# Four early expert slots, a bare last down, and the router of nine tiles moved from TensorE to VectorE

## What is computed

```
q, k, v: (4, 8, 576, 64)       # 2304 tokens in all, d_model 512
attn = softmax(masked(q @ k.T / 8)) @ v            # heads 0-3 local, 4-7 strided
x  = attn as (2304, 512)
xn = x / sqrt(mean(x * x) + 1e-6) * rms_g
y  = (silu(xn @ w_gate) * (xn @ w_val)) @ w_out    # d_ff 1536
logits = y @ router_w + modality_bias[modality_id] # 8 experts
e_idx  = argmax(logits); gate = softmax(logits)[e_idx]
for e in range(8):
    rows = (e_idx == e)
    out[rows] = gate[rows] * (relu(y[rows] @ w1[e]) @ w2[e])   # 512 -> 1024 -> 512
```

## Time and profile before

| | us |
|---|---|
| median of 3 runs | 913.56 (911.46 to 914.18) |
| the profiled execution | 913.16 |
| its span | 911.3 |
| start of chunks 1 to 5 (evacuation of y before) | 160.9, 257.5, 359, 455.3, 535.8 |
| start of the expert part | 617.5 |
| start of up(4), the first step of the steady loop | 678.4 |

### The profile page before, as it was taken

One profiled execution on the slowest core, in us unless ns is written; L12 is line 12 of the kernel. 1 busy time (PEld: TensorE's weight loads), 2 busy tenths in 40 slices (PEclk: granted clock), 3 DMA queues, 4 the chain that ended last, 5 costly groups with the idle time before them and its releaser, 6 DMA issues.

```text
span 911.3 us, 15931 instructions
## 1 busy us (share of the span) xinstructions
PE 888.4 (97%) x5407; PEld 760.2 (83%) x5407; DVE 443.2 (49%) x1239; ACT 363.9 (40%) x935; POOL 314.2 (34%) x371
## 2 busy tenths in 40 slices
PE   9989999999999999999999999999889999999995
PEld 5667898888888888899999999998678888888884
DVE  5864555333443335422522344774674467446651
ACT  6866413545454444521221131232262345335530
POOL 2734772334323343245234323240511122211221
PEclk9989999999999999999999999999899999999998
DMA  8982212222114210211121121610846365415511
GB/s 184 278 193 78 52 52 64 76 66 75 50 43 111 61 36 25 70 35 36 47 70 35 47 70 36 231 47 36 308 162 226 133 220 187 179 69 185 202 55 36
DMA packets 74486, 94.95 MB, mean 104 GB/s; under 512 B 38701, under 2 KB 42797, under 8 KB 74416
## 3 DMA queue, kind: packets, MB, share of 16 engines
q1 hardware_dynamic: 70656, 82.51, 29.8%
q0 software_dynamic: 3760, 11.54, 3.7%
HBM read 84.59 MB, written 10.22 MB: 104 GB/s over the span
## 4 chain that ended last, share of the span: by engine, by line
PE 91%; DVE 3%; issue 2%; POOL 1%; ACT 1%; DMA 1%; SPq 0%; ACTq 0%; DVEq 0%; POOLq 0%
PE ps L1130 34%; PE ps L1169 16%; PE ps L1621 12%; PE ps L1636 12%; PE ps L1061 3%; PE ps L1090 3%; PE ps L1071 2%; PE ps L1206 2%; PE ps L1037 2%; PE ps L1648 2%; PE ps L1199 1%; PE ps L587 1%; PE ps L1189 1%; DMA w_raw<-in_moe_w 1%; DVE w_lo L1785 1%
## 5 line engine op out<-in xcount | busy, mean ns | idle before, releaser
L1463 DVE SCALAR_TENSOR_TENSOR h<-h,ps 128x384 f32<-128x384 f32 x72 | 39.8, 553 | 151.8 <-ACT h L1321 151.8
L924 POOL TENSOR_TENSOR sm<-sm,rinv 72x288 f32<-72x288 f32 (+1 forms) x51 | 45.5, 893 | 193.8 <-DVE rinv L1407 193.7
L1130 PE MATMUL ps<-x_hi,val_hi 128*128 128x384 f32 x288 | 100.9, 350 | 0.0
L1130 PE MATMUL ps<-x_hi,gate_hi 128*128 128x384 f32 x288 | 100.9, 350 | 0.0
L954 POOL CAST out_hi<-out_raw 128x512 fp32r<-128x512 f32 x72 | 47.1, 655 | 149.3 <-DMA out_raw<-in_moe_w_out 149.3
L956 POOL TENSOR_TENSOR out_lo<-out_raw,out_hi 128x512 fp32r<-128x512 f32 x72 | 95.8, 1330 | 5.8
L1130 PE MATMUL ps<-x_hi,gate_lo 128*128 128x384 f32 x288 | 97.3, 338 | 0.0
L1130 PE MATMUL ps<-x_hi,val_lo 128*128 128x384 f32 x288 | 96.6, 335 | 0.0
L1130 PE MATMUL ps<-x_lo,val_hi 128*128 128x384 f32 x288 | 96.4, 335 | 0.0
L1130 PE MATMUL ps<-x_lo,gate_hi 128*128 128x384 f32 x288 | 94.1, 337 | 0.0
L1325 ACT ACTIVATE h_hi<-h 128x384 fp32r<-128x384 f32 x72 | 37.8, 525 | 130.9 <-DVE h L1469 130.9
(11 more groups left out here) (248 smaller groups left out, 1908.6 us busy)
## 6 DMA issues: line engine op xcount, KB each, us to landing
w_raw<-in_moe_w SPq DMA_DIRECT2D x64, 512.0 KB, 6.6
out_raw<-in_moe_w_out SPq DMA_DIRECT2D x72, 256.0 KB, 2.6
x_rows<-y_tiles SPq DMA_DIRECT2D x18, 256.0 KB, 2.4
early_w_raw<-in_moe_w SPq DMA_DIRECT2D x8, 512.0 KB, 6.3
gate_raw<-in_moe_w_gate SPq DMA_DIRECT2D x4, 768.0 KB, 10.0
val_raw<-in_moe_w_val SPq DMA_DIRECT2D x4, 768.0 KB, 10.1
qk<-in_q SPq DMA_DIRECT2D x8, 288.0 KB
qk<-in_k SPq DMA_DIRECT2D x8, 288.0 KB
```

The lines of the kernel that those rows point to most:

```text
L924: pool.tensor_tensor(s3, s3, rinv[0:n, i, :].unsqueeze(2).to_broadcast([n, 4, c]), ALU.mult).then_inc(s_no, 1)
L1130: mm = pe.matmul(ps[:, bank, 0:CH], w[:, i, kk, cols], x[:, kk, :], start=(m == 0), stop=(m == n - 1))
L1463: dve.scalar_tensor_tensor(out=hf[n % 2][:, :], in0=hf[n % 2][:, :], scalar=1.0, in1=ps[:, 0, 0:CH], op0=ALU.add, op1=ALU.mult).then_inc(s ...
```

## The change

**Four early slots.** `EARLY_SLOTS` is 4: the two fullest experts of the first 15 tiles get two slots each. `early_expert` finds both (19 small instructions on DVE where there were 11), `early_ranks` and `early_marks` rank within both. The second one's weights are issued by SP in `second_weights`, when the last gate product is done and ahead of the store of the last chunk. Rows of slots 2 and 3 are gathered from the first 15 tiles, right after the last y is evacuated. The order of steps on all engines is written anew: the placement stands behind down(1) and turn_h(2), and turn_rows(4) in the middle of down(2).

**Nested steps and a last down of its own.** The optional steps are nested `If`s (`while_live`), each for t up to the number of slots, and `last(s, n_used)` has only the last down: ACT copies hT_hi in two halves, DVE makes hT_lo in two, TensorE takes all high terms first and then the low ones. POOL's waits for open transfers stand ahead of its last scatter.

**Logits by DVE.** The nine tiles of chunks 0 to 2 are neither turned nor multiplied on PE. SP loads the router onto all partitions (2 MB written, `ROUTER`), ACT copies it apart by expert (`rw_of`), SP reloads each tile of y from `x2` (`y_again`), and DVE computes each of the 72 dot products of a tile and an expert as one multiply-and-sum of 128x512 (`dot`), three in five ticks from f = 5 of chunk 3 to the start of chunk 5. The compiler makes two instructions of it, the product and the read of its sum.

```diff
-EARLY_SLOTS, EARLY_TILES = 2, NTT - TT
-SB = NTT + E - 2
+EARLY_SLOTS, EARLY_TILES = 4, NTT - TT
+SB = NTT + E - 3
...
-for c in range(NC - 2):
+for c in range(NC - 3, NC - 2):
...
+DOTTED = TT * (NC - 3)
+ROUTER = at(NC - 3, 4, 0)
+DOT = {(i, e): at(NC - 3, 5, 0) + (E * i + e) * 5 // 3 for i in range(DOTTED) for e in range(E)}
+DOT_AT = by_tick((k, s) for k, s in DOT.items())
+DOTTED_AT = by_tick((i, DOT[i, E - 1] + 1) for i in range(DOTTED))
+RELOAD_AT = by_tick((i, DOT[i, 0] - 8) for i in range(DOTTED))
+BY_EXPERT_AT = by_tick((e, DOT[0, e] - 1) for e in range(E))
...
-        STEPS = SLOTS + 2
+        s_hi_a = sem("last_hT_hi_first_half")
+        s_lo_a = sem("last_hT_lo_first_half")
+        s_ilast = sem("last_scatter_index")
+        s_last = sem("last_rows_scattered")
+
+        STEPS = SLOTS + 1
         AHEAD = 3
-        SURE = NTT + 2
+        SURE = NTT + 1
         w1v = w1.rearrange("e (t p) n -> e p t n", p=P)
         w2v = w2.rearrange("e (t p) n -> e p t n", p=P)
         last_row = []
         route_steps = [0]
 
-        def run(eng, step):
-
-            with eng.Fori(0, (SURE - 4) // 4) as i:
+        def while_live(eng, n_used, do, t=None):
+
+            t = SURE if t is None else t
+            if t < STEPS:
+                with eng.If(n_used > t - 1):
+                    do(t)
+                    while_live(eng, n_used, do, t + 1)
+
+        def run(eng, step, last):
+
+
+            whole = (SURE - 5) // 4
+            with eng.Fori(0, whole) as i:
                 for n in range(4):
-                    step(4 * i + 4 + n, n)
-            n_used = eng.value_load(used[0:1, 0:1], min_val=0, max_val=SLOTS)
-            for t in range(SURE, STEPS):
-                with eng.If(n_used > t - 2):
-                    step(t, t % 4)
-            return n_used
+                    step(4 * i + 5 + n, (5 + n) % 4)
+            for t in range(5 + 4 * whole, SURE):
+                step(t, t % 4)
+            n_used = eng.value_load(used[0:1, 0:1], min_val=NTT, max_val=SLOTS)
+            s = eng.value_load(final[0:1, 0:1], min_val=NTT - 1, max_val=SLOTS - 1)
+            while_live(eng, n_used, lambda t: step(t, t % 4))
+            last(s, n_used)
...
+            for i, count in enumerate((count_1, count_2)):
+                of = star[:, i, :]
+                link(dve, dve.tensor_reduce(most[:, i:i + 1], count[:, :], axis=AX, op=ALU.max))
...
+        def second_weights(sp):
+
+            sp.wait_ge(s_g, FT * NC)
+            sp.sem_inc(s_f1, 1)
+            sp.sem_inc(s_f2, 1)
+            e = sp.value_load(star_i[0:1, 1:2], min_val=0, max_val=E - 1)
+            load(sp, e, 2, w1r, w1v, s_w1, s_f1)
+            load(sp, e, 2, w2r, w2v, s_w2, s_f2)
...
+                if s == ROUTER:
+                    sp.wait_ge(s_oe, G)
+                    sp.dma_start(rw_all[:, :, :].rearrange("p d e -> p (d e)"),
+                                 router_w.rearrange("d e -> (d e)").partition_broadcast(P)).then_inc(s_rwa, 16)
+                for i in RELOAD_AT.get(s, []):
+                    if i >= 3:
+                        sp.wait_ge(s_ld, i - 2)
+                    sp.wait_ge(s_x2, 16 * TT * (i // TT + 1))
+                    sp.dma_start(y_again[i % 3][:, :], x2[i * P:(i + 1) * P, :]).then_inc(s_ya[i % 3], 16)
...
+            second_weights(sp)
             store(NC - 1)
...
+                for e in BY_EXPERT_AT.get(s, []):
+                    act.wait_ge(s_rwa, 16)
+                    act.activation(rw_of[e][:, :], rw_all[:, :, e], ACT.Copy).then_inc(s_rwe, 1)
...
+            def dot(i, e):
+
+                if e == 0:
+                    dve.wait_ge(s_ya[i % 3], 16 * (i // 3) + 16)
+                if i == 0:
+                    dve.wait_ge(s_rwe, e + 1)
+                if E * i + e:
+                    dve.wait_ge(s_dot, E * i + e)
+                if e == 0 and i >= 2:
+                    dve.wait_ge(s_ld, i - 1)
+                dve.tensor_tensor_reduce(out=unread[:, :], in0=y_again[i % 3][:, :], in1=rw_of[e][:, :], scale=1.0,
+                                         scalar=0.0, op0=ALU.mult, op1=ALU.add,
+                                         accum_out=dots[:, i % 2, e:e + 1]).then_inc(s_dot, 1)
+
+            def add_bias_to_dots(i):
+                if i == 0:
+                    dve.wait_ge(s_bu, 6)
+                dve.wait_ge(s_dot, E * i + E)
+                dve.tensor_tensor(logit[:, i, :], dots[:, i % 2, :], bias_t[:, i, :], ALU.add).then_inc(s_ld, 1)
...
+            pool.wait_ge(s_ye, NC)
+            gather(pool, 2, 2)
+            gather(pool, 3, 3)
...
+            def last(s, n_used):
+
+                pool.tensor_copy(idx_last[:, :], idx_scatter[:, bass.ds(s, 1)]).then_inc(s_ilast, 1)
+                pool.wait_ge(s_ilast, 1)
+                for n in range(4):
+                    pool.wait_ge(s_xg[n], 16 * len(range(n, SURE + AHEAD, 4)))
+                for n in range(2):
+                    pool.wait_ge(s_out[n], 16 * len(range(n, SURE - 2, 2)))
+                while_live(pool, n_used, arrived)
+                pool.wait_ge(s_yo, s + 1)
+                pool.nop(nofuse=True)
+                pool.indirect_dma_start(out=out[:, :],
+                                        out_offset=bass.IndirectOffsetOnAxis(ap=idx_last[:, 0:1], axis=0),
+                                        in_=yo_last[:, :], in_offset=None,
+                                        bounds_check=last_row[0], oob_is_err=False).then_inc(s_last, 16)
+
+            run(pool, step, last)
+            pool.wait_ge(s_last, 16)
...
             turn_h(0)
-            up(1, range(KT // 2))
-
+            up(1, [0])
             pe.wait_ge(s_hot, 2)
             pe.matmul(ps[:, 2, 0:NTT * E], upper[:, :], hot_b[:, :, :], start=True, stop=True)
             pe.matmul(ps[:, 6, 0:NTT * E], ones_b[:, :], hot_b[:, :, :], start=True, stop=True).then_inc(s_cnt, 1)
-            up(1, range(KT // 2, KT))
+            up(1, range(1, KT))
+            turn_rows(pe, 2, 2)
             down(0)
             turn_h(1)
+            up(2)
+            turn_rows(pe, 3, 3)
+            down(1)
+            turn_h(2)
             pe.wait_ge(s_car, 6)
             pe.wait_ge(s_pay, 2)
             for i in range(NTT):
@@ -1685,11 +1814,11 @@
                                payload[:, i, :, :].rearrange("p a s -> p (a s)"),
                                start=(i == 0), stop=(i == NTT - 1))
             mm.then_inc(s_pl, 1)
-            down(1)
-            turn_rows(pe, 2, 2)
-            up(2)
-            turn_rows(pe, 3, 3)
-            turn_h(2)
+            up(3)
+            down(2, range(FJ // 2))
+            turn_rows(pe, 4, 0)
+            down(2, range(FJ // 2, FJ))
+            turn_h(3)
...
+            def last(s, n_used):
+
+                pe.wait_ge(s_hi_a, 1)
+                pe.wait_ge(s_yo, s)
+                for j in range(FJ):
+                    if j == FJ // 2:
+                        pe.wait_ge(s_hth, s + 1)
+                    if j % 2 == 0:
+                        pe.wait_ge(s_w2l, PIECES * s + j // 2 + 1)
+                    for w in (e2h, e2l):
+                        pe.matmul(ps[:, 5, :], hTh[:, j, :], w[:, j, :], start=(j == 0 and w is e2h), stop=False)
+                pe.wait_ge(s_lo_a, 1)
+                for j in range(FJ):
+                    if j == FJ // 2:
+                        pe.wait_ge(s_htl, s + 1)
+                    mm = pe.matmul(ps[:, 5, :], hTl[:, j, :], e2h[:, j, :], start=False, stop=(j == FJ - 1))
+                mm.then_inc(s_yp, 1)
...
+            def last(s, n_used):
+                act.wait_ge(s_ht, s + 1)
+                act.wait_ge(s_yp, s)
+                act.activation(hTh[:, 0:FJ // 2, :].rearrange("p j n -> p (j n)"), ps[:, 3, :],
+                               ACT.Copy).then_inc(s_hi_a, 1)
+                act.activation(hTh[:, FJ // 2:FJ, :].rearrange("p j n -> p (j n)"), ps[:, 4, :],
+                               ACT.Copy).then_inc(s_hth, 1)
+                split(s, e2h, w2r, s_w2, s_w2h)
...
+            def last(s, n_used):
+                dve.wait_ge(s_hi_a, 1)
+                dve.tensor_tensor(hTl[:, 0:FJ // 2, :].rearrange("p j n -> p (j n)"), ps[:, 3, :],
+                                  hTh[:, 0:FJ // 2, :].rearrange("p j n -> p (j n)").bitcast(f32),
+                                  ALU.subtract).then_inc(s_lo_a, 1)
+                dve.wait_ge(s_hth, s + 1)
+                dve.tensor_tensor(hTl[:, FJ // 2:FJ, :].rearrange("p j n -> p (j n)"), ps[:, 4, :],
+                                  hTh[:, FJ // 2:FJ, :].rearrange("p j n -> p (j n)").bitcast(f32),
+                                  ALU.subtract).then_inc(s_htl, 1)
+                split(s, e2h, e2l, w2r, s_w2h, s_w2l, s_f2)
+                dve.tensor_copy(gate_last[:, :], gate_slot[:, bass.ds(s, 1)]).then_inc(s_gc, 1)
+                dve.wait_ge(s_gc, s)
+                dve.wait_ge(s_yp, s + 1)
```

(3 more changed lines are left out.)

235 lines of the change are left out of this document (146 added, 89 removed).

## The result

| | us |
|---|---|
| changed kernel, median of 4 runs | 900.86 (896.80 to 903.12) |
| kernel before, same chip | 912.92 |
| ratio, 95% interval | 0.9863 (0.9822 to 0.9905) |
| profiled execution, its span | 902.19, 899.3 |

The forecast was 890.1 with a range of 883.5 to 897.0. Both are above the range; 23 us were promised, 12 to 15 came.

A forecast was written before the change was run, and what follows sets the result against it. TensorE, busy for 97% of the span, was taken as the bound. Gains of 10.6 + 6.6 + 3.4 + 2.5 = 23.1 us took the profiled span from 911.3 to 888.2, about 890.1 us measured, range 883.5 to 897.0.

The forecast's parts named there:

- Part 1: Dense part: nine tiles' logits leave TensorE, 11.7 us less 0.6 and 0.5, a gain of 10.6 us (6 to 11.7).
- Chunk ends: Multiply-and-sums ahead of h and h_lo delay the last down half at two chunk ends: 0.3 us each, 0 to 3.
- The trace agrees only in part: Claim that a DVE operation beside POOL was slowed, 0.61 to 1.32 us, but not held for POOL's full 2.0 us.
- Rival A: POOL's out split holds the products in full: 0.6 to 1.4 us per chunk end, hand-over 0.6; 892.4 us, chance 0.15.
- I cost at nothing: Chunk 5: the eight small instructions that early_expert gains on DVE were taken to cost no time.
- The 0.5 us for the broadcast: Chunk 3: the 2 MB router transfer just fits before TensorE needs the scaled gate; 0.5 us lost, 0 to 4.
- Part 2: Hand-over from dense part to experts: 8.5 us of waits and low clock go, 1.9 come; gain 6.6 us (3 to 9).
- Part 3: Last step: the unused slot's up goes, 11.5 less 5.6 of down and 2.5 of wait; gain 3.4 us (2 to 5.2).
- Rival C: The jump over unrun steps' code costs 2 us in the last wait, the end gives nothing; 894.6 us, chance 0.12.
- Part 4: End of the span: POOL's remaining branches and waits move ahead of the last scatter; gain 2.5 us (0 to 5.4).
- part 5: Slot count: 21 slots in either kernel, so nothing lost or won.
- D, DVE as the bound: DVE bounds 20 f's from chunk 3's f = 5, slower than before; 940 us at 2.0 us per product, chance 0.04.

The follow-up runs named there:

- e10: Changed kernel with TensorE's jump to the last step's code ahead of the last turn of h instead of behind it; 894.94 us, ratio 0.9819.
- e3: Changed kernel without GpSimd's subtraction for out_lo from chunk 3 on, which alters the result and used 22 slots; 904.88 us, ratio 0.9928.
- e8: Changed kernel with each reloaded y tile copied by ACT to PSUM for DVE's multiply-and-sums, their places moved a little; 894.52 us, ratio 0.9807.
- e7: Changed kernel with DVE normalising the next chunk's x ahead of the h_lo beside it instead of behind; 892.90 us, ratio 0.9793.
- e17: Changed kernel measured once more, unchanged, as a control (also called changed again); 897.56 us, ratio 0.9835.
- e1: Changed kernel with the logits of all 15 early tiles on TensorE as before, so no multiply-and-sums on DVE; 905.33 us, ratio 0.9928.
- e2: Changed kernel with the 72 multiply-and-sums four or five in a row behind h_lo, none at chunk ends; 904.53 us, ratio 0.9915.
- e12: Changed kernel with the edits of e8, e7, e10 and e4, multiply-and-sums four per step, and chunk 5's early routing spread; 887.00 us, ratio 0.9728.
- e4: Changed kernel with DVE's branch for the w2 split ahead of the two hT_lo halves in the last step; 898.40 us, ratio 0.9854.
- e11: Changed kernel with the last down in its old form, whole hT_hi and hT_lo and no high terms first; 897.95 us, ratio 0.9823.
- e14: Changed kernel with the last-step edits of both e10 and e4; 894.94 us, ratio 0.9824.

## Why the prediction was wrong

**Part 1, 10.6 us forecast, 2.1 measured: the failed part.** In the six profiles with this code it gave 2.0 to 5.7 us, 5.7 where the clock never fell (e10), so the draw of the clock explains part of the gap and the mechanism the larger part. The work taken off TensorE was sized right: chunk 2 fell by 3.8, and chunk 3 by 3.9 wherever nothing was held. Four things were missed.
- *Chunk ends, "I take 0.3 us for each", 0.6 in all.* Measured: 3.6 and 1.5 us (2.0 and 1.1 in e10). The product between h and h_lo cost little. The ones ahead of h were held by GpSimd (e3, e8), and at chunk 4's end they were too many even at 0.69 us (1.1 us in e8). The estimate of 0.61 us for one start to the next was low too: 0.73, of which the product is 0.68.
- *"The trace agrees only in part": the misreading behind it.* The product at 641.17 took 1.32 us beside a GpSimd operation from 640.00 to 642.03. I compared lengths, 1.32 with 2.03. Ends tell it: 642.49 is GpSimd's end plus 0.46, so most of the product's own 0.61 us came behind it. It had been held in full. Rival A, built on the rule of the Trainium skill, "SBUF — State Buffer", section on who interferes with whom, had the mechanism right and the price too low: it counted 0.6 to 1.4 us for a chunk end and had neither the late start of everything behind nor the clock.
- *Chunk 1, no term at all.* TensorE waits 1.6 us for x (0.6 before), as the router's work no longer covers DVE's normalise. e7 shows it. Another 1.5 us of this one execution were a low clock behind that wait; e17 took 100.8.
- *Chunk 5, "I cost at nothing".* 1.9 us, without any multiply-and-sum up to 3.5 (e1): the placement waits 0.7 for at_pos and two products 0.8 for h, and in eight of fourteen profiles the clock falls behind the placement.

The 0.5 us for the broadcast was not needed: it was issued at 393.00 and ready for ACT 7.4 us later, and TensorE did not wait.

**Part 2, 6.6 forecast, 7.9 measured: right in its mechanism, near in its sum partly by luck.** The waits and the low clock lost their place as said. up(0) to up(4) went from 60.9 to 51.6, 9.3 less, more than all of the 8.5 that the forecast counted. up(2) waited 0.17 where 1.3 was feared, and up(4) 0.58 as forecast. The placement itself, at full clock, fell from 3.42 us to 2.19, a term that was missing. Then the first down in the steady loop waits for w2, also missing, and up(4) to the last turn takes 1.4 longer:

```profile
639.09 0.70 PE L1746 MATMUL ps<-w_hi,xg_hi 128*128 128x512 f32 x2 [0.17 <-DVE w_lo L1985]
...
651.87 2.19 PE L1813 MATMUL ps<-payload,at_pos 128*128 128x92 f32 x18
...
667.08 0.72 PE L1746 MATMUL ps<-w_hi,xg_hi 128*128 128x512 f32 x2 [0.58 <-DVE xg_lo L648]
686.80 0.47 PE L1761 MATMUL ps<-w_hi,hT_hi 128*128 128x512 f32 x1 [1.15 <-DVE w_lo L1952]
```

**Part 3, 3.4 forecast, 0.4 measured: the sum was incomplete.** The wait of 2.5 us was 2.16. The stall of 1.54 us behind it and 1.4 us of slow clock were not in it. Rival C had named the jump to code that is far away; I gave it 0.12 and let the steady loop's steps of 12.40 us speak against it, which say nothing about a jump out of the loop. The Trainium skill, "Runtime: NRT & Kernel Launch", section on instruction fetch, says that a taken branch out of the fetched window stalls; it gives no length. These runs agree as far as a stall behind such a jump goes, with 3.3 to 4.3 us from the turn's end to the second matmul.

**Part 4, 2.5 forecast, 1.6 measured; part 5, 0: right** (21 scatters). Part 4 was half of its bound by guess: from the scatter's landing to the end are now 4.3 us instead of 5.4, where the forecast expected 3, and the landing itself took 2.7 instead of 3.2. **D, DVE as the bound,** did not happen in the changed kernel, but e2 came near to it: DVE busy 13.54 of 15 us from 475 us on, chunk 4 8.7 us longer than before. **The sum:** 2.1 + 7.9 + 0.4 + 1.6 = 12.0, which is 911.3 - 899.3. One more fault runs through it: only part 2 counted the clock behind a wait, where the earlier trace rows showed 0.87. The new waits of parts 1 and 3 had none.

## What to carry to other kernels

Before work goes to DVE, look at its operands: in these traces two in SBUF made DVE and GpSimd one engine with one budget, and one in PSUM took the work out of it. To see whether an operation was held, compare its end with the other's end, not its length. A pause of half a microsecond to two was followed by a lower clock in some executions and not in others, and cost up to 1.7 us more when it was; so give a new wait a range with that at its end, and compare a stage over several profiles before its time is put down to an edit. And put a jump to far code ahead of work that is already queued, not behind it.

## What the runs showed of the hardware

- 72 of 72 multiply-and-sums with one operand in PSUM took 0.678 to 0.693 us beside GpSimd or not; with both in SBUF, 0.676 to 1.780, and all 29 over 0.70 ended 0.54 to 0.56 us behind the end of a GpSimd operation. In all traces, gate scaling and h (one operand in PSUM) took 0.54 to 0.56 us beside GpSimd too. GpSimd is held in its turn: out_lo 1.28 us alone, 1.62 behind a multiply-and-sum.
- Small operations are held as well: an addition of 8 columns with both operands in SBUF took up to 0.83 us (e2) and 1.23 us (changed kernel) instead of 0.16.
- A pause of 0.46 to 0.67 us ahead of 15 small matmuls was followed by a lower granted clock in eight of fourteen profiles (0.69 over 5 us in e12). One of 1.85 us ahead of a down was followed by about 3 us at the lower level, and ones of 1.69 to 1.77 us at the same place in five other profiles (changed again, e4, e10, e11, e14) by none. Which pause brings the clock down is open.
- Behind the jump to the last step's code the second matmul came 3.3 to 4.3 us after the turn (12 kernels); with the turn behind the jump, 1.8 to 2.5 (4 kernels).
